# Placing the weight tiles and the activation tiles of an fp32r MoE kernel at one residue modulo 4096 bytes

## What is computed

```
logits = x @ w_gate ; noisy = logits + log1p(exp(x @ w_noise)) * noise
h = max(x[mask] @ w1[e], 0) ; out[mask] += weight * (h @ w2[e])      # two experts per token
h = x @ w_in ; out = (h - tanh(h)) @ w_out                           # dense part
```

## The kernel before, in words

| tile | start | modulo 4096 | modulo 512 |
|---|---|---|---|
| w_hi0, w_lo0, w_raw0, w_raw1 | 16512, 49280, 82048, 90240 | 128 | 128 |
| ident | 98432 | 128 | 128 |
| blocks | 98944 | 640 | 128 |
| w_hi1, w_lo1 (and q_sb) | 99072, 131840 | 768 | 256 |
| idx_g, idx_s | 164608, 164640 | 768, 800 | 256, 288 |
| y2, x_hi, x_lo, h_hi, h_lo, y_sb | 164672, 172864, 176960, 181056, 197440, 213824 | 832 | 320 |
| u_sq, th, large, g32 | from 217920 | 832 or 2880, g32 3392 and 1344 | 320 (large 320) |
| c_w0, c_w1 | 228672, 228832 | 3392, 3552 | 320, 480 |

## Time and profile before

### The profile page before, as it was taken

One profiled execution on the slowest core, in us unless ns is written; L12 is line 12 of the kernel. 1 busy time (PEld: TensorE's weight loads), 2 busy tenths in 40 slices (PEclk: granted clock), 3 DMA queues, 4 the chain that ended last, 5 costly groups with the idle time before them and its releaser, 6 DMA issues.

```text
span 2150.3 us, 36878 instructions
## 1 busy us (share of the span) xinstructions
PE 1961.3 (91%) x13280; PEld 1756.8 (82%) x13281; DVE 1051.3 (49%) x2002; ACT 836.5 (39%) x1776; POOL 562.8 (26%) x527
## 2 busy tenths in 40 slices
PE   5865776199999999999999996999999999999999
PEld 5655665198989899899899895898899988999888
DVE  6755564331313131313131313777667776677765
ACT  4544554232323132323132322544444444444444
POOL 3244432412121121121121212222222322232222
PEclk9988899599999999999999998999999999999999
DMA  8343331331313131313131313000010000110000
GB/s 218 103 116 100 92 93 34 102 118 54 123 54 122 40 135 39 117 59 117 39 112 63 114 61 117 31 30 29 29 56 32 29 29 29 46 42 29 29 29 20
DMA packets 79077, 152.34 MB, mean 71 GB/s; under 512 B 12768, under 2 KB 37472, under 8 KB 76224
## 3 DMA queue, kind: packets, MB, share of 16 engines
q1 hardware_dynamic: 62720, 108.42, 16.2%
q0 software_dynamic: 16320, 43.45, 6.0%
HBM read 111.51 MB, written 40.33 MB: 71 GB/s over the span
## 4 chain that ended last, share of the span: by engine, by line
PE 83%; DVE 7%; another core or an unknown queue 4%; issue 2%; DMA 2%; ACT 1%; POOL 0%; DVEq 0%; SPq 0%; ACTq 0%; POOLq 0%
PE banks L705 13%; PE banks L707 13%; PE banks L706 13%; PE banks L696 12%; PE banks L697 12%; PE banks L698 12%; PE banks L686 3%; PE banks L593 2%; DVE kp L1014 1%; PE banks L612 1%; PE banks L572 1%; DMA v_raw<-in_v 1%; DVE mx L1025 1%; PE banks L581 1%
## 5 line engine op out<-in xcount | busy, mean ns | idle before, releaser
L696 PE MATMUL banks<-x_hi,w_hi 128*128 128x256 f32 x2304 | 640.0, 278 | 5.3 <-DVE x_lo L1224 4.1
L697 PE MATMUL banks<-x_lo,w_hi 128*128 128x256 f32 x2304 | 639.7, 278 | 0.0
L698 PE MATMUL banks<-x_hi,w_lo 128*128 128x256 f32 x2304 | 639.2, 277 | 0.0
L705 PE MATMUL banks<-w_hi,h_hi 128*128 128x512 f32 x1184 | 471.7, 398 | 3.0 <-DVE h_lo L1248 3.0
L707 PE MATMUL banks<-w_hi,h_lo 128*128 128x512 f32 x1184 | 467.2, 395 | 0.0
L706 PE MATMUL banks<-w_lo,h_hi 128*128 128x512 f32 x1184 | 466.3, 394 | 0.0
L696 PEld LDWEIGHTS banks<-x_hi,w_hi 128*128 128x128 f32 x2304 | 434.2, 188 | 8.5 <-DVE x_lo L1224 4.9
L697 PEld LDWEIGHTS banks<-x_lo,w_hi 128*128 128x128 f32 x2304 | 434.1, 188 | 2.2
L698 PEld LDWEIGHTS banks<-x_hi,w_lo 128*128 128x128 f32 x2304 | 433.7, 188 | 0.0
L534 POOL TENSOR_SCALAR large<-u_sq 128x512 uint8<-128x512 f32 x144 | 222.4, 1545 | 590.7 <-ACT u_sq L963 323.0
L1231 DVE SCALAR_TENSOR_TENSOR h_lo<-banks,h_hi 128x512 fp32r<-128x512 f32 x144 | 99.6, 692 | 386.9 <-ACT h_hi L914 259.2
(11 more groups left out here) (141 smaller groups left out, 2250.2 us busy)
## 6 DMA issues: line engine op xcount, KB each, us to landing
w_raw<-in_moe_w SPq DMA_DIRECT2D x32, 1024.0 KB
y<-y_rows SPq DMA_DIRECT2D x18, 1024.0 KB, 4.9
k_raw<-in_k SPq DMA_DIRECT2D x32, 288.0 KB
q_sb<-in_q SPq DMA_DIRECT2D x32, 288.0 KB, 4.1
v_raw<-in_v SPq DMA_DIRECT2D x8, 1152.0 KB
x_rows<-x_sb SPq DMA_DIRECT2D x32, 288.0 KB, 3.5
out_x<-y_sb SPq DMA_DIRECT2D x36, 256.0 KB, 2.1
w_raw<-in_moe_w_in SPq DMA_DIRECT2D x4, 1024.0 KB
```

The lines of the kernel that those rows point to most:

```text
L696: pe.matmul(part, hi, x_hi[:, c, :], start=(c == 0), stop=False)
L697: pe.matmul(part, hi, x_lo[:, c, :], start=False, stop=False)
L698: mm = pe.matmul(part, lo, x_hi[:, c, :], start=False, stop=(c == NC - 1))
L705: pe.matmul(p_y[m][:, :], hi, w_hi[par][:, o:o + DM], start=(j == 0), stop=False)
```

## The change

Only the order in which tiles are made is changed; no instruction, loop, wait or transfer is added or removed.

```diff
+        ident = sb("ident", [128, 128])
+        blocks = sb("blocks", [1, 4 * E], i32)
         w_hi = [sb("w_hi0", [128, WE], f32r)]
         w_lo = [sb("w_lo0", [128, WE], f32r)]
         w_raw = [sb(f"w_raw{i}", [128, WC]) for i in range(2)]
-        ident = sb("ident", [128, 128])
-        blocks = sb("blocks", [1, 4 * E], i32)
...
         w_hi.append(sb("w_hi1", [128, WE], f32r))
         w_lo.append(sb("w_lo1", [128, WE], f32r))
-        idx_g = sb("idx_g", [128, SUB], i32)
-        idx_s = sb("idx_s", [128, SUB], i32)
         y2 = sb("y2", [128, SUB, 2 * DM])
...
         g32 = [sb(f"g32_{i}", [128, 2 * NB]) for i in range(2)]
+        idx_g = sb("idx_g", [128, SUB], i32)
+        idx_s = sb("idx_s", [128, SUB], i32)
         c_w = [sb(f"c_w{i}", [128, TC]) for i in range(2)]
```

## The result

The changed kernel takes 2122.39 us (median of 4 runs, 2120.06 to 2123.16) against 2103.45 us for the kernel before on the same chip. The ratio is 1.0087, 95% interval 1.0073 to 1.0101. It was forecast to be faster.

The account below looks back on a forecast made before the run. TensorE's matmul start-to-start pace was taken as the bound behind the attention part. Odd blocks 11.0, half blocks 0.4 and dense downs 7.3 us saved gave -18.7, so 2102.5 became 2084 us; range 2048 to 2131.

Parts of the forecast that it names:

- everything put at nothing: Attention part (1 us allowed either way), small tiles, DMA, transposes, VectorE and ScalarE: new tile starts cost 0 or almost nothing.
- Two levels that depend on placement: TensorE matmuls: weights at 128 or 256 modulo 512 differ by 4.4 ns in up, 4.1 to 4.4 in down.
- slow everywhere: Bounding case for the matmul stream: every up and down matmul at the slower observed pace, +26.6 us.
- I take the fast level: Matmuls with weights and tokens both at 256: all run at the faster observed pace, -18.7 us; chance 0.38.
- The down seam: End of an odd block: last down matmul moves w_hi1 (256) while w_hi1 (256) loads; 0.23 us, read as fast.
- The up seam: End of an even block's up product: x_hi (320) moves while h_hi (320) loads; 0.11 us, read as fast.
- the case of the other sign: Whole kernel gets slower instead of faster: chance 0.38, so the range was taken up to 2131 us.
- The split answer: Matmul stream: downs at the fast level, ups at the slow one; +11.9 us, 2114 us; chance 0.08.
- Closer is slower: Even blocks and dense ups: pace falls as weights and tokens lie nearer modulo 512; +26.6 us, 2129 us; chance 0.30.
- No effect: Matmul levels come from something else that differs between parities and stays unchanged; 2102 us; chance 0.10.

Follow-up runs that it names:

- Downs equal, ups apart: Against the kernel before: all weights and h moved to 128 modulo 512, x at 320, small tiles as filler; ratio 1.0027.
- the two halves: Each half alone against the kernel before: all weights to 256, ratio 1.0116; y2, x, h, y_sb to 256 with weights left at 128 and 256, ratio 1.0106.
- the shift run: The changed kernel with 64 bytes put ahead of the weights, so weights, x and h all lie at 320 modulo 512; ratio 1.0100 to the kernel before.

## Why the prediction was wrong

**Bound, waits and everything put at nothing: right.** TensorE's border waits stayed (29.4 us both times, and 13.8 against 14.1). Nothing else became the bound; the net of the matmul paces (+18.1 us) is the measured change.

**Two levels that depend on placement: right for the down product, half right for the up product.** They reproduced at once when only the weights were moved, and the price of "slow everywhere", worked out from the trace at 26.6 us, measured 25. But that each placement has one pace in the up product held for this kernel only: the pair that ran at 113.3 ns in it ran at 117.8 in others ("Downs equal, ups apart"), with the same residues modulo 512. It did not cause the miss, since difference 0 gave 120.0 at every entry.

**The failed step: "I take the fast level" for the new combination.** It holds for neither product. Down: equal residues gave 226.7 ns, 2.3 below the fast level of 229; the sign was right and the gain was undersized (-19.1 us in all downs, where I had 7.3 for the dense ones and some 4 for the odd). Up: 120.0 ns, 6.6 above the fast level and above even the slow one. Ups are 6912 of 10464 matmuls, and they set the sign. The reason for the step was two seams, one matmul each. The down seam (0.23 us after 0.24) pointed the right way, but one step could not carry it: in the kernel before single settled steps run from 0.225 to 0.232 us in the even down phase and from 0.230 to 0.236 in the odd one. The up seam, `x_hi` 320 against `h_hi` 320 at 0.11 us, did not: a matmul in the seam still has the pace of the ones before it, and the steady pace of that same difference is 120.0. The changed kernel's own starts show how long settling takes: its first up steps are 0.11 and 0.12 us (424.17, 424.28, 424.40) before it is at 120. I had called these hints and then let them choose. That 2122 us lies between the forecast's 2048 and 2131 owes nothing to the step: the range was drawn wide to take in the case of the other sign.

**The rivals.** The split answer (downs fast, ups slow; chance 0.08, 2114 us) was the right shape: both its signs hold, and both levels lie beyond those that I had seen, so that it came out at +18.9 in place of +11.9. "Closer is slower" had the right total sign and a wrong mechanism, since it wanted slow downs. "No effect" is refuted by the result and by the run that moved the weights alone. With the same instructions, clock and work, the dense up product went from 113.3 to 120.0 ns as bytes moved. The Trainium skill ("SBUF — State Buffer", section "Who interferes with whom") says that TensorE's two read ports are independent and that TensorE waits for nobody. What I drew from it, that no byte address matters, does not hold here; the measurement decides. The runs do not show whether ports, banks or something else stands behind it.

**Shown, and open.** Shown: placement alone makes the measured loss, through 120.0 ns ups and 226.7 ns downs at difference 0 (the two halves, the shift run, and the sum of +18.1 us against +18.9). The down product follows the difference modulo 256, each pace seen at two or more pairs of starts. The up product's state at entry picks among several paces (the 0.60 us wait inside a product, the two paces in one trace, and the added transpose, none with a byte moved). Not shown: that the up product follows the difference alone for values other than 0, and that 512 bytes is the full unit for it. Open: what in the memory makes some differences costly, why the down product repeats at 256 and the up product does not, and which property of the entry does the picking.

## What to carry to other kernels

When two streams of back-to-back fp32r matmuls with the same shapes run at paces a few per cent apart, compare the starts, not the durations, and look at the byte addresses modulo 512 of what is loaded and what is moved; a common residue helped the 512-column product and hurt the 256-column one, so each product needs its own choice. Judge a placement by a settled stretch, never by the single step at a seam, and look at the product behind the one you improve: here ups behind downs of 226.7 ns ran at 117.8 in place of 113.3 until the entry was changed. If a pair settles at two paces in one trace, try a cheap odd matmul ahead of the product, and measure it: here it gave 1.1% in one layout, took 0.8% in another, and one transpose more undid the gain.

## What the runs showed of the hardware that was not expected

- fp32r matmuls of 128 x 256 with a new stationary slice each ran at 113.3, 116.7, 117.3, 117.4, 117.8, 118.7 or 120.0 ns from start to start, those of 128 x 512 at 226.7, 229, about 233 or 233.3 ns, all at the full granted clock (1.00 over 1450 to 2000 us in every trace). The placement made these paces, in the up product together with how it was entered.
- One layout and one instruction stream can settle at two paces (113.3 and 117.8 ns) in the same execution. One extra transpose ahead of a product of 96 or 192 matmuls, or one wait of 0.60 us inside it, changed which.
- At difference 0 the up product's LDWEIGHTS is recorded 5 ns longer (193 against 188 ns mean, in the changed and in the shifted kernel); the transposes (about 109 ns from start to start in every trace) did not react to any placement.
- The kernel before took 2103 us on two chips and 2150 to 2151 on two others; some 50 us of it lie ahead of the expert part.
